# A fifth place for x, in memory that the attention matrix fills later, and another order of the first loads

## What is computed

```python
# attention between 512 tokens and 32 state rows, for 8 batches x 8 heads, D = 64
a = softmax(scale * x @ state.T);   xread = a @ state
a2 = softmax(scale * state @ x.T);  sread = a2 @ x
x = concat([xread, sread])          # -> 4608 tokens of 512
# soft mixture: 8 experts x 4 slots, F = 1024
logits = x @ phi
d = softmax(logits, over tokens);   slot_input = d.T @ x
slot_out = relu(slot_input @ w1[e]) @ w2[e]
x = softmax(logits, over slots) @ slot_out
# one expert for each token
e = argmax(x @ w_gate)
out = gate * sigmoid(x @ w_output_gate)[e] * (relu(x @ w1[e]) @ w2[e])
```

## Time and profile before

| | |
|---|---|
| median of three runs | 483.99 us (481.11 to 485.51) |
| profiled execution, time | 480.1 us |
| profiled execution, span | 478.4 us |
| TensorE busy, matmuls | 425.4 us (89%) |
| VectorE busy | 141.5 us (30%) |
| ScalarE busy | 123.9 us (26%) |
| GpSimd busy | 123.7 us (26%) |
| moved by DMA | 87.27 MB, mean 182 GB/s |
| mean granted TensorE clock | 0.98 |

### The profile page before, as it was taken

How to read it: one execution, slowest core, us unless ns; L and a number is a source line. 1 busy time by engine, 2 the same in 40 slices (tenths; PEclk the granted TensorE clock), 3 DMA queues, 4 the chain that set the end, 5 groups by cost and what they waited for, 6 DMA issues and landing times.

```text
span 478.4 us, 9544 instructions
## 1 busy us (share of the span) xinstructions
PE 425.4 (89%) x3474; PEld 225.0 (47%) x3475; DVE 141.5 (30%) x381; ACT 123.9 (26%) x329; POOL 123.7 (26%) x191
## 2 busy tenths in 40 slices
PE   6879787699887757999999999999999999999991
PEld 5667564464324424544444444444444444444440
DVE  2589799850000870211111111010101010111100
ACT  3877675221000200212121212121212121211200
POOL 2343342104000003132323232323323232323110
PEclk9999999989899988999999999999999999999997
DMA  8989909759999999777665010101010110101110
GB/s 283 297 273 309 347 22 318 251 194 428 429 430 425 426 425 393 265 275 252 221 224 198 25 47 23 47 23 47 23 47 29 42 39 30 45 25 45 25 47 2
DMA packets 31710, 87.27 MB, mean 182 GB/s; under 512 B 6140, under 2 KB 14908, under 8 KB 29628
## 3 DMA queue, kind: packets, MB, share of 16 engines
q1 hardware_dynamic: 27580, 76.66, 43.4%
q0 software_dynamic: 3952, 9.54, 6.0%
q10 hardware_dynamic: 144, 0.59, 0.3%
HBM read 77.27 MB, written 9.78 MB: 182 GB/s over the span
## 4 chain that ended last, share of the span: by engine, by line
PE 72%; DMA 15%; DVE 6%; issue 3%; ACT 2%; POOL 1%; SPq 0%; POOLq 0%; DVEq 0%; ACTq 0%
PE bank L879 52%; DMA parts<-in_moe_w 11%; PE bank L866 5%; DMA arena<-in_x 4%; PE bank L763 3%; PE bank L551 2%; PE bank L540 2%; PE bank L564 1%; PE bank L781 1%; PE bank L581 1%; PE bank L859 1%; PE bank L700 1%; PE bank L592 1%; DVE rmx L1081 1%; PE bank L814 1%
## 5 line engine op out<-in xcount | busy, mean ns | idle before, releaser
L879 PE MATMUL bank<-arena,z 128*128 x560 | 249.4, 598 | 0.0
L879 PEld LDWEIGHTS bank<-arena,z 128*128 128x128 f32 x560 | 103.6, 190 | 121.7 <-issue 117.7
L1338 DVE TENSOR_SCALAR z<-bank 128x256 f32<-128x256 f32 x70 | 26.4, 419 | 218.1 <-PE bank L866 218.1
L1043 ACT ACTIVATE z<-bank,gate_to 128x512 f32<-128x512 f32 x35 | 24.0, 687 | 221.7 <-PE bank L879 221.7
L490 POOL DMA_INDIRECT out<-z,rows_to x35 | 36.1, 1033 | 29.9 <-POOL rows_to L487 29.9
L487 POOL CAST rows_to<-gate_to 128x1 int32<-128x1 f32 x35 | 6.4, 184 | 140.6 <-ACT z L1043 140.6
L470 POOL DMA_INDIRECT z<-token_rows,rows_from x32 | 33.6, 1049 | 25.6 <-POOL rows_from L477 25.6
L866 PEld LDWEIGHTS bank<-cT,z 32*128 32x128 f32 x560 | 18.8, 185 | 16.6 <-issue 16.4
L866 PE MATMUL bank<-cT,z 32*128 32x128 f32 x560 | 25.4, 296 | 0.0
L1035 ACT ACTIVATE z<-bank 128x256 f32<-128x256 f32 x70 | 23.0, 388 | 0.6 <-PE bank L866 0.6
L470 POOL DMA_INDIRECT z<-token_rows,sidx x4 | 4.2, 1055 | 69.8 <-DVE sidx L1316 68.9
(11 more groups left out here) (207 smaller groups left out, 397.1 us busy)
## 6 DMA issues: line engine op xcount, KB each, us to landing
arena<-in_moe_w SPq DMA_DIRECT2D x18, 2048.0 KB, 15.3
arena<-in_moe_w SPq DMA_DIRECT2D x32, 512.0 KB, 7.0
parts<-in_moe_w SPq DMA_DIRECT2D x6, 2048.0 KB, 18.2
arena<-in_x SPq DMA_DIRECT2D x7, 1024.0 KB, 8.2
arena<-in_x SPq DMA_DIRECT2D x2, 512.0 KB, 5.6
token_rows<-z ACTq DMA_DIRECT2D x1, 578.0 KB
out<-z,rows_to POOLq DMA_INDIRECT x35, 3.0
z<-in_state SPq DMA_DIRECT2D x1, 512.0 KB, 4.0
```

Of the source, the lines that this page charges most:

```text
L879: mm = e.matmul(pY[p][:, :], hT[p][:, c, :], arena[:, bass.ds(at * UNIT + 512 * c, 512)], start=(c == 0), stop=(c == CF - 1))
L1043: e.activation(ysb[p], pY[p][:, :], ACT.Copy, scale=gate_to[:, q, 0:1])\
L1338: v = e.tensor_scalar(hT[p][:, 2 * g:2 * g + 2, :], bank[g][:, 0:GW].rearrange("p (c t) -> p c t", c=2), 0.0, None, ALU.max)
```

## The change

A fifth place for x is made of columns 6144 to 8191 of `parts`, which `A` needs only for batches 6 and 7. `X_AT` maps the batches to the places: 0 to 4 have one each, and 5, 6 and 7 follow 0, 1 and 2. So x 1 to 4 are issued without a wait, x 5 waits until the slots of batch 0 have been read (`rd_psum` of 1), x 6 for 2 and x 7 for 3. GpSimd's multiplication for batches 6 and 7 waits for `rd_psum` of 5, since batch 4's x lies where it writes. The queue's order changes: unit 0 and the gate weights follow x 4, then x 5, unit 1, x 6, unit 2, x 7, unit 3, then the state pieces and the write of the first table rows. Unit 4 takes slot 4, and units 5 and 6 slots 6 and 7; unit 4 waits for `st_psum` of 16, unit 5 for `rd_psum` and `x_laid` of 7. The bytes moved and the arithmetic stay the same.

```diff
+X_AT = [0, 1, 2, 3, 4, 0, 1, 2]
-SLOT = [0, 1, 2, 5, 6, 4, 7, 3] + [8, 9, 0, 1, 2, 5, 6, 4] + [7, 3, 8, 9, 0, 1, 8, 9]
+SLOT = [0, 1, 2, 5, 4, 6, 7, 3] + [8, 9, 0, 1, 2, 5, 6, 4] + [7, 3, 8, 9, 0, 1, 8, 9]
...
-        x_sb = [arena[:, 6 * UNIT + 2048 * q:6 * UNIT + 2048 * (q + 1)] for q in range(4)]
+        x_sb = [arena[:, 6 * UNIT + 2048 * q:6 * UNIT + 2048 * (q + 1)] for q in range(4)] + [parts[:, 6144:8192]]
...
-            e.wait_ge(x_in[b % 4], 16 * (b // 4 + 1))
+            e.wait_ge(x_in[X_AT[b]], 16 * (b // 5 + 1))
...
-            e.tensor_copy(to, x_v[b % 4]).then_inc(x_laid, 1)
+            e.tensor_copy(to, x_v[X_AT[b]]).then_inc(x_laid, 1)
...
             def load_x(b):
-                if b >= 4:
-                    e.wait_ge(rd_psum, b - 3)
-                    e.wait_ge(x_laid, b - 3)
+                if b >= 5:
+                    e.wait_ge(rd_psum, b - 4)
+                    e.wait_ge(x_laid, b - 4)
...
-            for b in range(1, 4):
+            for b in range(1, 5):
                 load_x(b)
+            load_w(0)
+            e.dma_start(wg_sb[:, :, 0:NE], wgate.rearrange("(p c) e -> p c e", p=P)).then_inc(gates_in, 16)
+            e.dma_start(wg_sb[:, :, NE:2 * NE], wogate.rearrange("(p c) e -> p c e", p=P)).then_inc(gates_in, 16)
+            load_x(5)
+            load_w(1)
+            load_x(6)
+            load_w(2)
+            load_x(7)
+            load_w(3)
+            for i in range(2):
+                load_state(e, i)
             e.wait_ge(no_row_ready, 2)
             e.dma_start(table[0:FIRST_ROW, :], no_row[:, :]).then_inc(table_out, 16)
-            e.dma_start(wg_sb[:, :, 0:NE], wgate.rearrange("(p c) e -> p c e", p=P)).then_inc(gates_in, 16)
-            e.dma_start(wg_sb[:, :, NE:2 * NE], wogate.rearrange("(p c) e -> p c e", p=P)).then_inc(gates_in, 16)
-            load_w(0)
-            load_x(4)
-            load_w(1)
-            load_x(5)
-            load_w(2)
-            for i in range(2):
-                load_state(e, i)
-            load_x(6)
-            load_w(3)
-            load_x(7)
-            e.wait_ge(rd_psum, NB - 2)
-            e.wait_ge(x_laid, NB - 2)
+            e.wait_ge(st_psum, 2 * NB)
             load_w(4)
-            e.wait_ge(st_psum, 2 * NB)
+            e.wait_ge(rd_psum, NB - 1)
+            e.wait_ge(x_laid, NB - 1)
             load_w(5)
...
                     e.wait_ge(rr_ready, m + 1)
+                    if b >= 6:
+                        e.wait_ge(rd_psum, 5)
...
-                                          e2[i][:, j, NS * g:NS * g + NS], x_v[b % 4][:, 2 * g + i, j, :],
+                                          e2[i][:, j, NS * g:NS * g + NS], x_v[X_AT[b]][:, 2 * g + i, j, :],
```

More of the change, by code:

```diff
@@ L190, in build @@
         small_in, phi_in, rows_in = sem("small_in"), sem("phi_in"), sem("rows_in")
-        x0_in, x0_laid, x_in = sem("x0_in"), sem("x0_laid"), [sem(f"x_in{q}") for q in range(4)]
+        x0_in, x0_laid, x_in = sem("x0_in"), sem("x0_laid"), [sem(f"x_in{q}") for q in range(5)]
         w_in, w_used = [sem(f"w_in{q}") for q in range(NE + 2)], sem("w_used")
@@ L329, in load_x @@
             def load_x(b):
-                if b >= 4:
-                    e.wait_ge(rd_psum, b - 3)
-                    e.wait_ge(x_laid, b - 3)
-                e.dma_start(x_sb[b % 4].rearrange("p (h c) -> p h c", h=NH),
-                            x[b].rearrange("h (p j) d -> p h (j d)", j=J)).then_inc(x_in[b % 4], 16)
+                if b >= 5:
+                    e.wait_ge(rd_psum, b - 4)
+                    e.wait_ge(x_laid, b - 4)
+                e.dma_start(x_sb[X_AT[b]].rearrange("p (h c) -> p h c", h=NH),
+                            x[b].rearrange("h (p j) d -> p h (j d)", j=J)).then_inc(x_in[X_AT[b]], 16)
             def load_w(u):
```

## The result

The changed kernel takes 476.7 us (median of 20 runs, 475.71 to 479.89), the kernel before 482.18 (median of 20, 479.95 to 485.55). The ratio is 0.9895, with a 95% interval of 0.9871 to 0.9919: about 5.1 us faster, 3.9 to 6.2. That gap between the medians and the two profiles is what the experiments had to explain.

A forecast was written before the change was run, and what follows sets the result against it. The prediction took a fixed-length weight stream, started when the attention stage ends, as the bound; VectorE paces that stage's steps. 484.0 less 2.3 us from two x steps gave 481.7, range 478.6 to 486.0.

The forecast's parts named there:

- a microsecond arrives whole: Attention stage, 0 to 103.8 us: each microsecond gained there starts the fixed-length weight stream earlier and reaches the end in full.
- the steps fall to VectorE's pace: Attention loop: both waits for x 6 and x 7 go, and their steps of 10.22 and 9.37 us become 8.64.
- 1.58 + 0.73 = 2.3: Attention loop: microseconds gained in the steps of x 6 and x 7, from 10.22 and 9.37 down to 8.64.
- The bound of 4.0 us: Attention loop: most the x steps could gain, TensorE's idle time of 2.57 + 1.47, if a step could be under 8.64.
- The base: Whole kernel: starting time from which the gain was subtracted, the 484.0 us median of three runs.
- (A): Rival near 31 to 34 us: TensorE's code arrives later behind added load, up to 3.4 us, giving 485.1; chance 0.20.
- (D): Rival ahead of line 700: one low-clock stretch more or less, 1.5 us, giving 480.2 or 483.2; chance 0.12.
- (B): Rival before 103.8: gain spent on a late x or GpSimd's copy meeting VectorE's two-port work; no change, 484.0; chance 0.13.
- (C): Rival in attention stage: steps fall by 4.0 us and the 33.55 stall vanishes with its 1.4, giving 478.6; chance 0.10.
- What was costed at nothing: State pieces, gate weights, first table rows, GpSimd's new wait, units 4 to 7, slot exchange: all covered or hidden, no cost.
- sign of being wrong: End of attention stage: unit 7 landing after line 700 has ended was listed as evidence against the forecast.
- 3 us of cover: Queue before the attention matrix is free at 101.5: some 3 us idle, beyond which a late unit 7 delays unit 8.

The follow-up runs named there:

- e10: Kernel of e4 with more empty transposes at the end of the attention stage; 475.88 us against 481.71 of the kernel before, ratio 0.9884.
- e6: Changed kernel with the state pieces put back ahead of x 7 and unit 3; 477.97 us against 482.95 of the kernel before, ratio 0.9893.
- e4: Changed kernel with units 0 to 3 issued later, unit 0 behind x 6; 476.51 us against 482.13 of the kernel before, ratio 0.9891.
- e9: Kernel before, still four places, but x 4 and 5 ahead of unit 0, x 6 and 7 ahead of units 1 to 3; 476.28 us against 481.71, ratio 0.9907.
- e11: Kernel of e4 unchanged, run again for a second profile; issue into `parts` at 98.3 to 100.0 us among the four profiles without early units.
- e15: Kernel before unchanged, its seventh profile; profiled time 483.05 us.
- e7: Kernel before unchanged, its third profile; profiled time 482.69 us.
- e1: Kernel before unchanged, its second profile; profiled time 480.75 us.
- e13: Kernel before unchanged, its fifth profile; profiled time 480.52 us.

## Why the prediction was right or wrong

**What bounds the kernel, and that a microsecond arrives whole: right, with an exception.** In all eleven profiles of the two kernels the last unit lands 83.8 to 84.1 after the issue into `parts`, and the span ends 290.7 to 290.8 after that. In e10 1.5 us of the gain were lost behind the landing, in e6 1.0.

**The waits for x go and the steps fall to VectorE's pace: right.** 8.53 each against the 8.64 forecast. (In the step of 8.64 GpSimd did wait for x 5; the step after x 7, with no x to wait for, takes 8.53.) x 6 and x 7 landed at 41.1 and 52.5; forecast were 40.4 to 43.8 and 47.6 to 51.0. x 7 was 1.5 us later than that and still in time. But in the late steps it is TensorE and not VectorE that sets the length: its busy time and its wait fill them.

**The size of that term, 1.58 + 0.73 = 2.3: this step failed.** It was right for the execution it was read from, where the two steps exceeded 17.06 by 2.5. Over seven executions the excess is 3.2 in the mean and up to 5.5. What the term left out is TensorE's clock: the wait was priced at the clock of that execution, and in three of seven the clock fell in or just behind it, which made TensorE's matmuls in the step of x 6 2.7, 1.6 and 1.5 us longer, 0.8 in the mean. Without that the excess is 2.3, the number forecast. The wait itself varied too (1.74 to 3.66 us), as the queue holds x 6 back until 44.7 to 47.8. The bound of 4.0 us, TensorE's idle time, was no upper bound, since it too came from that execution and had no term for the clock. The steps explain 3.2 of the 3.6 us between the profiles. Of the 5.1 between the timed runs 1.5 stay unexplained.

**The base.** The forecast of 481.7 stood on the median of three runs, 484.0. Twenty runs give 482.2, and from there the same 2.3 us would have given 479.9. So the base accounts for 1.8 of the 5.0 us by which the forecast was too high, and the size of the gain for 3.2.

**(A), code later: its sign appeared.** A stall of 1.67 us at 24.46 appeared in the profiled run, one of 1.4 or more in three of four profiles. What the stalls cost more is smaller than the waits that went, so the gain never turned into a loss. e4, e9, e10 and e11 show that they go with the early load, not that the code is what comes late. The rule of the Trainium skill (Runtime: NRT & Kernel Launch, "Instruction fetch mechanics") that the fetch is mostly hidden agrees with the four profiles without early units, which had no stall near 24 or 33; of the 14 with them it agrees with 4.

**(D), the clock: looked for in the wrong place.** It was priced at 1.5 for the end of the stage. There one stretch costs 1.6, in five of seven profiles of before (twice that in e15) and two of four of the changed kernel, and in the mean the two kernels differ by only 0.3 us in that part. What distinguishes them is the fall in or behind the wait for x 6.

**(B) and (C).** (B) did not happen. (C) gave 478.6, the nearest number, by luck: its stall did not vanish, and its 4.0 us for the steps is not the 3.2 measured.

**What was costed at nothing stayed at nothing.** The state pieces (47.67 to 57.66), GpSimd's new wait, units 4 to 7 and the slot exchange show nowhere in the time. Unit 7, though, was forecast to land by 98 and did not: its last piece left at 92.7 and landed 9.2 later, at 101.9, as line 702 ended. That is the sign of being wrong that the prediction had named. It cost nothing that can be seen, since the last unit landed 84.0 after the issue as in the others, but the 3 us of cover were gone.

**What stays open.** The timed runs are about 5.1 us apart by the ratio, the profiled executions 3.6. With seven and four profiles this can be chance. No execution of before above 483.05 was profiled, while timed ones reach 485.6, and 486.9 beside the experiments. Of the 44 executions timed there, the 12 above 483 had a mean granted clock of 0.963 and the 11 below 481 one of 0.973, so the slow ones spend longer at the low level. Where, was not seen. A long wait with a fall of the clock on top of a code stall, as in e7, would do it, but this is argued and not shown.

## What to carry to other kernels

Before pricing a wait, read it in several executions. The price of a late transfer in a step is the wait of the engine behind it, less what that engine has to spare in a step without one, plus what it loses in speed. Here that was 0.85 to spare, and up to 2.7 us lost to TensorE's clock. A load that a loop step needs should not stand in its queue behind bulk loads and many small pieces that nobody needs for another 50 us; here putting x first gave the x steps with four places what the fifth place gave them. The gap between two single profiles is not the gain: here it was 1.9 us where the timed runs lay 5.1 apart, because stalls and stretches at the low clock come and go.

## What the runs showed of the hardware

- The granted clock fell to 0.50 inside a wait of 3.66 us, for 6.8 us, and the step took 14.02 and not 8.53 us (e1). It fell 0.5 us behind a wait of 2.54 (e13) and 1.6 behind one of 3.15 (e7). Beside waits of 2.50, 2.57, 2.70 and 1.74 us in the same place it did not fall.
- TensorE stopped 1.4 to 2.9 us, for nothing that the profile shows, in the middle of unrolled matmuls in 10 of 14 profiles with bulk loads early in the queue, and in none of the four without.
- Issuing the same eight state pieces occupied the queue for 7.8 us in the first profile, 10.2 in e1, 10.0 in the changed kernel and 15.4 in e9.
